# Attention with its keys on the partitions: the maximum as a row of the contraction, float32 probabilities, no engine loops

## The reference

```python
q_rot, k_rot = rotate(q), rotate(k)                # by cos and sin of the position
scores = scale * q_rot @ k_rot.T                   # 576 x 576 for each of 32 heads
attn = exp(scores - max(scores, axis=-1))
attn = attn / (sum(attn, axis=-1) + 1e-9)
x = (attn @ v)                                     # -> [2304, 512]
h = x @ w_in1;  x = (h - tanh(h)) @ w_out1
h = x @ w_in2;  out = (h * sigmoid(1.702 * h)) @ w_out2
```

## Time and profile before

| | us |
|---|---|
| median of 3 runs | 1217.45 |
| the profiled execution, from first to last instruction | 1217.3 |
| busy: PE, ACT, DVE, GpSimd | 1149.3, 582.7, 603.0, 235.3 |
| first score product starts | 19.77 |
| first product of the feed-forward layers starts | 406.79 |
| last ACT copy of the output starts | 1213.28 |

### The profile page before, as it was taken

The page is one execution under the profiler, slowest core; times in us unless marked ns, Lnnn a source line. Parts: engine busy times, 40 slices in busy tenths (PEclk is TensorE's granted clock), DMA queues, the critical chain, the costliest instruction groups (busy, mean ns, idle before and its releaser), DMA issues.

```text
span 1217.3 us, 19081 instructions
## 1 busy us (share of the span) xinstructions
PE 1149.3 (94%) x6640; PEld 1074.6 (88%) x6640; DVE 603.0 (50%) x1045; ACT 582.7 (48%) x1259; POOL 235.3 (19%) x227
## 2 busy tenths in 40 slices
PE   3889989998998899999999999999999999999998
PEld 3778878887887899999999999999999999999997
DVE  5878887888788664322323332345423232323222
ACT  3888887888888553222323222335422232223222
POOL 7475666656652000000000000000000000000000
PEclk9989998999999999999999999999999999999999
DMA  4223222322241343000000000025100000000000
GB/s 128 61 68 88 68 78 58 97 58 78 77 138 36 106 148 121 16 12 27 26 26 26 26 26 26 27 61 156 51 20 27 27 26 26 26 26 0 26 1 27
DMA packets 58603, 65.22 MB, mean 54 GB/s; under 512 B 9920, under 2 KB 47808, under 8 KB 58560
## 3 DMA queue, kind: packets, MB, share of 16 engines
q1 hardware_dynamic: 58560, 64.63, 17.6%
HBM read 41.03 MB, written 14.16 MB: 45 GB/s over the span
## 4 chain that ended last, share of the span: by engine, by line
PE 83%; ACT 7%; DVE 4%; issue 4%; DMA 1%; ACTq 0%; SPq 0%; POOL 0%; DVEq 0%; POOLq 0%
PE PS L592 32%; PE PS L612 16%; PE PS L609 16%; PE PS L515 6%; PE PS L534 5%; PE PS L547 5%; ACT probs L651 2%; ACT other_y L682 2%; ACT k_st L671 1%; DVE q_st L837 1%; DMA k_sw<-k_st 1%; DVE pt_lo L827 1%; ACT pt_hi L660 1%; PE PS L500 1%; ACT x_pair L681 1%
## 5 line engine op out<-in xcount | busy, mean ns | idle before, releaser
L592 PE MATMUL PS<-x_hi,w_parts 128*128 128x384 f32 x1536 | 422.8, 336 | 0.0
L923 DVE TENSOR_TENSOR g_raw<-PS,act_t 128x384 f32<-128x384 f32 x192 | 107.0, 558 | 391.7 <-ACT act_t L747 200.9
L592 PEld LDWEIGHTS PS<-x_hi,w_parts 128*128 128x128 f32 x1536 | 280.5, 188 | 4.2
L592 PE MATMUL PS<-x_lo,w_parts 128*128 128x384 f32 x768 | 257.2, 335 | 0.0
L609 PE MATMUL PS<-g_hi,w_parts 128*128 128x384 f32 x768 | 210.4, 334 | 0.4 <-DVE x_out L864 0.4
L612 PE MATMUL PS<-w_parts,g_hi 128*128 128x512 f32 x576 | 195.1, 393 | 1.0 <-DVE y_sb L938 0.8
L928 DVE TENSOR_TENSOR g_lo<-g_raw,g_hi 128x384 fp32r<-128x384 f32 x192 | 107.3, 559 | 114.8 <-ACT g_hi L754 114.8
L754 ACT ACTIVATE g_hi<-g_raw 128x384 fp32r<-128x384 f32 x192 | 100.8, 525 | 125.1 <-DVE g_raw L923 121.9
L747 ACT ACTIVATE act_t<-PS 128x384 f32<-128x384 f32 x96 | 47.2, 492 | 211.1 <-PE PS L592 211.1
L592 PEld LDWEIGHTS PS<-x_lo,w_parts 128*128 128x128 f32 x768 | 144.2, 188 | 4.1
L819 DVE TENSOR_REDUCE neg_max<-PS 128x1 f32<-128x576 f32 x160 | 120.3, 752 | 53.8 <-PE PS L515 53.3
(11 more groups left out here) (76 smaller groups left out, 1315.2 us busy)
## 6 DMA issues: line engine op xcount, KB each, us to landing
k_sw<-k_st SPq DMA_DIRECT2D x32, 288.0 KB, 3.7
x_raw<-x_scratch SPq DMA_DIRECT2D x12, 768.0 KB, 4.4
raw_w<-moe_w_in_dram SPq DMA_DIRECT2D x32, 256.0 KB, 2.9
raw_w<-moe_w_out_dram SPq DMA_DIRECT2D x32, 256.0 KB, 3.2
x_scratch<-x_out SPq DMA_DIRECT2D x16, 288.0 KB, 2.2
x_scratch<-y_sb SPq DMA_DIRECT2D x6, 768.0 KB, 3.5
raw_k<-k_dram SPq DMA_DIRECT2D x16, 256.0 KB, 2.7
raw_q<-q_dram SPq DMA_DIRECT2D x16, 256.0 KB, 2.9
```

The costliest lines, as they stand in the source:

```text
L592: last = nc.tensor.matmul(h_banks[j % 2], w_parts[:, j, w, c * P:(c + 1) * P], x[par][:, c, :], start=(c == 0 and w == 0 and x is x_hi), s ...
L923: nc.vector.tensor_tensor(g_raw[:, j % 2, :], h_banks[j % 2], act_t[:, j % 2, :], ALU.subtract if m == 0 else ALU.mult).then_inc(g_done, 1)
```

## The change

The attention is written anew, head by head, with straight-line code for all engines.

- Keys on partitions. `scores(h, t)` makes a tile of 128 keys by 576 queries, so the probabilities come out as the product with v wants them. They are not transposed, and not cut: `probs_v` multiplies float32 probabilities by float32 values (not float32r), 2 products of 288 columns a tile, 10 a head.
- The maximum. It is needed for each query, now a column. `near_scores` makes scores with queries on partitions for the next head from the high query part and both key parts (2 one-pass products of 288 columns a tile). DVE takes its row maximum, PE transposes the five columns of maxima into one row (`maxima_across`), ACT copies it into row 64 of `q_lm`. `k_h1` has ones there, so the product adds minus the maximum. The near scores round differently from the scores, and the same shift stands in the sum.
- The sums. `v_one` holds v in half of its columns and ones in the other; the product gives the sums in the other 64 partitions. One ACT copy a head takes both out (`copy_pv`). A row of sums goes by DMA to 9 columns of 64 partitions, DVE inverts, DMAs write it to DRAM and read it back on 64 partitions, GpSimd multiplies (`normalise`).
- Queries are transposed head by head (64 stationary columns), and ACT writes their high part twice, `q_hh`. A DMA copies the key's high half to `k_h1`. SP loads v straight into `v_one`, 256 bytes a piece. DVE's memsets at the start set ones and pads.
- PSUM: 3 slots of two banks in one ring for scores, near scores, keys, maxima rows and queries; 2 banks for the product with v. Probabilities have 5 buffers, the product runs 2 tiles behind the scores.
- The feed-forward layers compute as before. Weights are cut five chunks ahead in the first layer, five of them inside the attention; buffers that were shared with the attention are apart; unit loops are unrolled; the tokens are dealt back at the last store (two pieces for some tiles) and no longer by DVE; the first unit's second product isn't split.

```diff
-        score_slots = [PS[:, 2 * j:2 * j + 2, 0:HALF] for j in range(2)]
-        ring_banks = [PS[:, 4 + j, :] for j in range(RING_BANKS)]
-        pv_bank = PS[:, 7, 0:HALF]
+        slots = [PS[:, 2 * j:2 * j + 2, :] for j in range(SLOTS)]
+        pv_banks = PS[:, 6:8, 0:HALF]
...
+            def near_scores(h, t):
+                slot_free("M", h, t)
+                if t == 0:
+                    pe.wait_ge(q_hi_done, 2 * h + 2)
+                    pe.wait_ge(k_lo_done, h + 1)
+                slot = slot_halves(slot_of("M", h, t))
+                for b in range(2):
+                    last = nc.tensor.matmul(slot[:, b, :], q_hh[h % 2][:, t * P:(t + 1) * P],
+                                            k_hl[h // 2 % 2][:, h % 2, b * HALF:(b + 1) * HALF], start=True, stop=True)
+                last.then_inc(m_ready, 1)
+            def maxima_across(h):
+                slot_free("R", h)
+                pe.wait_ge(max_done, (h + 1) * TILES)
+                slot = slot_columns(slot_of("R", h), PADDED)
+                for i in range(TILES):
+                    last = nc.tensor.transpose(slot[0:1, i * P:(i + 1) * P], neg_max[h % 2][:, i:i + 1], ident[:, :])
+                last.then_inc(r_ready, 1)
+            def scores(h, t):
+                slot_free("S", h, t)
+                if t == 0:
+                    pe.wait_ge(q_lo_done, h + 1)
+                    pe.wait_ge(row_done, h + 1)
+                    pe.wait_ge(k_copied[h // 2 % 2], h // 4 * 16 + 16)
...
+                for b in range(2):
+                    nc.tensor.matmul(slot[:, b, :], k_hl[par][:, a, keys], q_hh[h % 2][:, b * HALF:(b + 1) * HALF],
+                                     start=True, stop=False)
+                for b in range(2):
+                    last = nc.tensor.matmul(slot[:, b, :], k_h1[par][0:HD + 1, a, keys],
+                                            q_lm[h % 2][0:HD + 1, b * HALF:(b + 1) * HALF], start=False, stop=True)
+            def probs_v(g):
+                h, t = divmod(g, TILES)
+                pe.wait_ge(exp_done, g + 1)
+                if t == 0:
+                    pe.wait_ge(loaded["v"][h // 2 % 2], h // 4 * 64 + 64)
+                    if h:
+                        pe.wait_ge(pv_copied, h)
+                for b in range(2):
+                    last = nc.tensor.matmul(pv_banks[:, b, :], v_one[h // 2 % 2][:, h % 2, t, :],
+                                            probs[g % PROBS][:, b * HALF:(b + 1) * HALF], start=t == 0, stop=t == TILES - 1)
+                last.then_inc(pv_done, 1)
+            for h in range(-2, NHEADS):
+                now, ahead = h >= 0, 0 <= h + 1 < NHEADS
+                for t in range(TILES):
+                    g = h * TILES + t - PV_LAG
+                    if now:
+                        scores(h, t)
+                    if ahead and t in (2, 3):
+                        near_scores(h + 1, t)
+                    if ahead and t == 3:
+                        near_scores(h + 1, 4)
+                    if t == 4 and h % 2 == 0 and h + 2 < NHEADS:
+                        keys_across((h + 2) // 2)
+                    if t == 4 and ahead:
+                        maxima_across(h + 1)
+                    if now and g >= 0:
+                        probs_v(g)
+                    if ahead and t in (0, 1):
+                        near_scores(h + 1, t)
+                if h + 2 < NHEADS:
+                    queries_across(h + 2)
...
+            for h in range(-2, NHEADS):      # ACT
+                for t in range(TILES):
+                    if h >= 0:
+                        exp(h, t)
+                    if t == 1 and h >= 1:
+                        copy_pv(h - 1)
...
+                if h % 2 == 0 and h + 2 < NHEADS:
+                    keys_hi(h + 2)
+                if 0 <= h + 1 < NHEADS:
+                    row(h + 1)
+                if h % 2 == 0 and h + 2 < NHEADS:
+                    keys_hi(h + 3)
+                if h + 2 < NHEADS:
+                    queries_hi(h + 2)
...
+            for h in range(-2, NHEADS):      # DVE
+                for t in range(TILES):
+                    if 0 <= h + 1 < NHEADS:
+                        row_max(h + 1, t)
...
+                if h % 2 == 0 and h >= 2:
+                    invert(h // 2 - 1)
+                if h % 2 == 0 and h + 2 < NHEADS:
+                    keys_lo(h + 2)
+                    keys_lo(h + 3)
+                if h + 2 < NHEADS:
+                    queries_lo(h + 2)
```

More of the change, by code:

```diff
@@ L50, with ring_order, out_pieces, stored_by @@
 CUT_AT = 8
[L57 to L72, removed]
+CUT_EARLY = 5
+APART = 4
+SLOTS = 3
+PROBS = 5
+PV_LAG = 2
+def ring_order():
+    order = []
+    for h in range(-2, NHEADS):
+        now, ahead = h >= 0, 0 <= h + 1 < NHEADS
+        for t in range(TILES):
+            if now:
+                order.append(("S", h, t))
+            if ahead and t < TILES - 1:
+                order.append(("M", h + 1, t))
+                if t == TILES - 2:
+                    order.append(("M", h + 1, t + 1))
+        if h % 2 == 0 and h + 2 < NHEADS:
+            order.append(("K", h + 2, 0))
+        if ahead:
+            order.append(("R", h + 1, 0))
+        if h + 2 < NHEADS:
+            order.append(("Q", h + 2, 0))
+    return order
+RING = ring_order()
+def out_pieces(tile):
+    pieces, col = [], tile * P
+    while col < (tile + 1) * P:
+        b, c = divmod(col, SEQ)
+        end = min((tile + 1) * P, b * SEQ + (min((c // P + 1) * P, SEQ)))
+        if c < FULL * P:
+            first, step = b * SEQ + c % P * FULL + c // P, FULL
+        else:
+            first, step = col, 1
+        pieces.append((col - tile * P, end - tile * P, first, step))
+        col = end
+    return pieces
+STORES = [1] * UNITS + [sum(len(out_pieces(u * UT + t)) for t in range(UT)) for u in range(UNITS)]
+def stored_by(n):
+    return 16 * sum(STORES[:n])
 def program(nc, q, k, v, w_in1, w_out1, w_in2, w_out2, cos_t, sin_t, out):
@@ L312, in store_y, with store_tile @@
+            fetch_sums(NHEADS - 1)
+            store_x(PAIRS - 2)
+            def store_tile(tile):
+                for first, last, row, step in out_pieces(tile):
+                    rows = bass.ds(row, last - first, step=step) if step > 1 else slice(row, row + last - first)
+                    sp.dma_start(out[rows, :], y_sb[first:last, tile % UT, :]).then_inc(y_stored, 16)
             def store_y(m, u):
@@ L453, in _, with slot_free @@
+            pool.wait_ge(consts_in, 32)
+            rope("k", 1)
+            rope("q", 1)
+            for pair in range(PAIRS):
+                if pair + 2 < PAIRS:
+                    rope("k", pair + 2)
+                    rope("q", pair + 2)
+                if pair:
+                    normalise(pair - 1)
+            normalise(PAIRS - 1)
         @block.tensor
         def _(pe):
-            def bank_free(pair, idx):
-                back, b = idx - RING_BANKS, pair
+            def slot_free(kind, h, t=0):
+                back = RING.index((kind, h, t)) - SLOTS
@@ L741, in nonlinear @@
                 act.wait_ge(h_ready, at + 1)
-                if not (isinstance(at, int) and at < 2):
+                if at >= 2:
                     act.wait_ge(g_done, at - 1)
@@ L751, in g_high @@
                 act.wait_ge(g_done, at + 1)
-                if not (isinstance(at, int) and at < STAGES):
+                if at >= STAGES:
                     act.wait_ge(out_done, at + 1 - STAGES)
@@ L820, in row_max @@
                                         negate=True).then_inc(max_done, 1)
-            def probs_lo(pair, a, c, idx):
-                dve.wait_ge(pt_hi_done, (pair * 2 + a) * CHUNKS + c + 1)
-                if c == 0 and not is_static(pair, 0):
-                    dve.wait_ge(pv_ready, pair * 4 + a * 2 - 2)
-                keys, queries, cols = parts_of_chunk(c)
-                nc.vector.tensor_tensor(pt_lo[a][:, keys, queries],
-                                        ring_banks[idx % RING_BANKS][:, 0:cols].rearrange("p (t n) -> p t n", t=keys.stop - keys.start),
-                                        pt_hi[a][:, keys, queries].bitcast(F32), ALU.subtract).then_inc(pt_lo_done, 1)
```

812 lines of the change are left out of this document (325 added, 487 removed).

## The result

| | before | after |
|---|---|---|
| median, us | 1218.07 (4 runs, 1216.74 to 1219.30) | 1189.10 (4 runs, 1188.25 to 1189.93) |
| first to last instruction in the profile, us | 1217.3 | 1186.5 |
| first score product starts | 19.77 | 21.01 |
| one pair of heads, steady laps | 23.8 to 23.9 | 22.25 |
| first product of the feed-forward layers starts | 406.79 | 376.15 |

The ratio is 0.9765, 95% interval 0.9749 to 0.9781: 29 us less, where the prediction said 9. The direction held, but not for the reason forecast: the prediction left the lap where it was (24.0 us for 23.8) and took its 9 us from the start and the end of the attention, while most of the measured gain lies in the laps.

What follows compares the result with a forecast made beforehand. PE's stream and waits were taken to bound the attention: 20.6 + 3.4 = 24.0 us a lap. Attention end 398.6 + later layers 803.6 + first-unit losses 2.0 + tail 4.6 = 1208.8; forecast 1208, range 1180 to 1246.

Steps and rivals of the forecast that it cites:

- The product: Attention's float32 product of probabilities and v, 288 columns: four passes with hidden loads, 0.493 us each, twenty 9.9 a pair.
- The transposes of the maxima: Ten a pair on PE, priced at 0.109 us each; the skill's load rule would make them 0.06.
- The waits of the new order: PE's waits in an attention lap: five terms, together 3.4 us, with hand-overs of 0.36 and 0.14 us.
- (1): Even head's end: the next S0 (score product) waits for key halves through ACT and DVE, 1.4 us late.
- (2): Odd head's end: S1 (score product) waits for query halves, low half and three hand-overs, 0.6 us.
- (3): At a head's end: M0 (near-score product) waits for the next query's halves, 0.5 us.
- (4): The maxima's transposes wait for DVE's fourth and fifth maximum: 0.35 us a head, 0.7 a lap.
- (5): PV (product with v) waits for the copy of the last one: 0.3 us a lap.
- Open loads: Rival: each float32 product's weight load, 0.109 us, is not hidden, 0.60 instead of 0.493; whole 1231 us, chance 0.20.
- Cheap product: Rival: a float32 product costs 0.245 us as by the transposes, lap 21.5; whole 1168 us, chance 0.12.
- Low clock: Rival: sparse PE work from keys' transposes to S0 brings back the lower clock, 28 us; whole 1236, chance 0.15.
- No movement: Rival: layout errors cancel the 9 us gain, whole 1215 to 1220 us, chance 0.10.

Runs made afterwards that it cites:

- run 7: Kernel with query transposes and second key half moved earlier, plus maxima, identity and target of the maxima's transposes as float32r: 1172.55 us, ratio 0.9631.
- run 4: Changed kernel with the exponential given back a zero bias tile and the unread accumulator of row sums: 1193.73 us, ratio 0.9803.
- run 2: Changed kernel with float32r probabilities times a constant tile in place of v, so a one-pass product: 1140.27 us, ratio 0.9375.
- run 3: Changed kernel with query transposes ahead of the last PV step and ACT's second key half ahead of the maximum row: 1173.34 us, ratio 0.9629.
- run 6: Changed kernel with only the query transposes moved ahead of the last PV step, ACT's order kept: 1178.37 us, ratio 0.9682.
- run 8: Changed kernel with four more unread ACT copies ahead of an even head's key halves, so S0 comes late: 1253.44 us, ratio 1.0295.
- run 1: Kernel before the change with its engine loops written out, arithmetic, queues and order kept: 1208.24 us, ratio 0.9923.

## Why the prediction was off

**The product (right, 2% high).** Four passes with hidden loads was the choice between 0.133 and 0.97, at 0.493; it measured 0.482, which is 4 x 0.120. The fixed 0.013 that was added does not appear. Twenty are 9.6 instead of 9.9, so the stream of a pair is 5.3 + 2.7 + 2.7 + 9.6 = 20.4, forecast 20.6. The float32 transpose was the wrong neighbour, as the prediction judged: there one instruction takes the time of two cycles of 2.4 GHz per column (0.109 for 128), and a product takes two such instructions (0.241 each for 288). "FP8 and Floating Point Precision", TensorE Precision Notes, in the Trainium skill has a count that fits this time (four passes of high and low parts), though the trace shows two instructions a product and no passes. The 0.53 that was estimated from it was 10% too much, because it charged four full products.

**The transposes of the maxima (right against the rule).** By "TensorE: Matmul & The Clock Gate", LDWEIGHTS, in the Trainium skill the prediction estimated them at 0.06 each, for their one stationary column. They stand (0.71 - 0.272) / 4 = 0.11 apart, as those of 128 columns, and run 7 halves that with the same one column, by the type of both operands. So the column count of the load did not set this pitch, the type did. (The 0.4 us a lap that the prediction put on the rule would have been 0.8 by its own 0.06 and 0.08.)

**The waits of the new order (the step that failed).** 3.4 us were laid out (the five terms as written add up to 3.5); the lap shows 22.25 - 20.4 = 1.85. Term by term, by the starts read above: (1) S0 is 0.97 late where 1.4 was laid out; (2) and (3) S1 and M0 are 0.56 and 0.10 late where 0.6 and 0.5 were; (4) and (5), 0.7 for the maxima and 0.3 for the copy of the product, are not there in a steady lap. The 0.2 left are the first two products behind each wait, which take 0.50 to 0.53 instead of 0.43. Keys first and queries second, and the engines they wait for, were right; the price of a hand-over was not. It was put at 0.36 us from the slot of PE's last product to the other engine's start and at 0.14 on the way back, both from the earlier trace rows, and both rows were misread:

- The bracket [0.20 <-PE PS L515] at 22.09 is DVE's idle time, not the distance to its releaser. DVE had ended at 21.89. PE's last product is this one, of the same timeline of the kernel before:

```profile
21.38 0.68 PE L515 MATMUL PS<-k_sw,q_st 128*128 128x288 f32 x2
```

  It ends at 22.06, 0.03 ahead of DVE's start. In the kernel after, the same shows on ACT:

```profile
201.03 0.43 PE L503 MATMUL PS<-q_lm,k_h 65*128 65x288 f32 x2
...
201.50 0.65 ACT L608 ACTIVATE probs<-PS 128x576 f32<-128x576 f32 x1 [1.06 <-PE PS L503]
```

  The product ends at 201.46 and the exponential starts 0.04 later, with 1.06 in its bracket. From the slot it is 0.29 - 0.13 + 0.04 = 0.20. (A matmul's end is modelled by the profiler. By starts alone, the last product's to the exponential's, it is 0.34, where the prediction's reading makes 0.49.)

- The 0.14 back to PE ran from the end of the exponential, at 22.67. Behind it stood the accumulator's read, which ended at 22.76: from there to PE's load at 22.81 it is 0.05.

The same layout with 0.20 and 0.06 gives 22.8; with the exponential at 0.651, 22.66; with the product at 0.482, 22.4 to 22.5. The 0.2 left is a wait for maxima that the layout has (step 4, 0.47 of it still) and the steady laps don't. So by this arithmetic, of the 1.75 us a lap 1.2 are the hand-over, 0.14 the exponential (run 4, with the accumulator's read, gives 0.17), 0.2 the product. This split is a layout by hand and no run; what the runs show is that forecasts with the corrected price came out (18.7 for 18.41 in run 2, where the old price gave 20.3, 21.2 for 21.12 in run 3 and 21.65 for 21.53 in run 6). Sixteen pairs at 1.75 are 28 us less than forecast.

**Start, ends and what follows.** The first score came at 21.0 (20.6 forecast). The layers behind the attention start at 376.15 (396 to 401 forecast); with the PV step inside them the attention ends at 377.1 by the prediction's count, where it had 398.6. That is 21.5 less, not 28: from the first score it is 356.1, as much as sixteen steady laps of 22.25, so the 6 us taken off for what the first and last heads don't have did not show. Laps that also cut weights take 2.9 of them (14 x 0.21), the ends 3.2. The layers' own time is 804.2 (805.6 forecast): the loss in the first unit is one stall of 0.78 us before the first L571 where 2.0 were charged. The tail is 5.1 (4.6), in which SyncE issues the last tile in six stores, 3.67 us, where before three took 1.64. The sum closes: 377.1 + 804.2 + 5.1 = 1186.4, the profile's 1186.5.

**Against which time.** The time of an execution is 1.8 us more than its span (1188.3 and 1186.5 after), so the one profiled before, with a span of 1217.3, was above its median of 1217.45. By spans the change is 30.8, by medians 29.0; "no shift" in the prediction neglected 1.8 us.

**Loads of the others.** A lap has ACT 13.68 (14.1 forecast, less the exponentials), DVE 11.98 (11.0), POOL 13.42 (12.5): all covered, as said. The chain of the sums never held ACT.

**The rivals.** Open loads (0.60 a product): refuted by 0.482. Cheap product: refuted by the same number, and run 2 puts its worth at 49 us at most. Low clock: 1.00 throughout; runs 2 and 8 show it alive at waits of 1.5 and 3.5 us. No movement: refuted. Of the prediction's "2.9 us more stream for 2.7 fewer us of waits, gaps and low clock" only the first half came out: 2.7 more stream, for 4.3 fewer, of which the low clock is some 1.7. That the time still lay in the range of 1180 to 1246 is partly luck: no case of the prediction had a lap of 22.25 us, and 1180 was chosen to stop above the cheap product.

Open: the 0.2 us a lap between layout and measurement is assigned to step (4) by the absence of its wait in the list, not by a run of its own; and why the first and last laps are 3.2 us longer than laid out was not tried.

## What to carry to other kernels

Price a hand-over from the releaser's end to the next start, in both directions, and look whether the releaser is the instruction you think; a bracket of idle time says only how long the engine had nothing to do. When a reordering puts a chain of small copies between two stretches of matmuls, that chain at the pair's end is the thing to lay out and to move: two moves of whole blocks were worth 16 us, more than half of what the rewrite gave. And a saving on PE counts only where PE isn't about to wait (run 7: 0.5 us a lap saved, nothing gained; run 2: half of it gained). Thinning PE's stream can also bring the low clock back (runs 2 and 8).

## What the runs showed of the hardware

- A float32 product of 288 columns is two instructions 0.241 us apart, 0.482 together: four times the 0.120 of one column per cycle of 2.4 GHz; a float32r product of 288 columns stands 0.133 from the next. A float32 transpose of 128 columns is one instruction at 0.11, whether it has 128, 64 or 1 stationary columns; in float32r it is 0.057 (run 7, both operands).
- An exponential of 128x576 from PSUM takes 0.651 us without bias tile and accumulator, 0.742 with them, and 0.193 more for the accumulator's read (run 4).
- From the recorded end of one engine's instruction to the start of the next engine's: 0.03 to 0.06 us, in the four places read (PE to DVE and ACT, DVE and ACT to PE). In a fifth, the queries' low half on DVE to S1 on PE, it is 0.14 (199.80 + 0.75 = 200.55 to 200.69).
- Written-out loops removed 28.9 us shown as issue and were worth 9.4 us, part of that by a clock that stayed up in more laps; the rest turned into other waits (run 1).
- After a gap of 3.52 us PE ran 4 us at 0.57 of full speed, 1.6 us lost, but not behind two of fifteen such gaps (run 8). With waits of 1.5 us a lap the lower clock came in five places, 1.2 us lost each time (run 2); with 0.80 us once a lap it lost nothing.
